# Attention on one core: the large score matmuls move directly behind the transposes, the small ones and the ninth block to the end of the step, and the ninth block into the second transposition bank

## The reference

```python
# q, k, v: (4, 8, 1152, 64)
q_pool = q.reshape(B, H, S // 2, 2, D).mean(axis=3)          # 576 queries of a head
scores = scale * np.matmul(q_pool, k.transpose(0, 1, 3, 2))  # 576 x 1152
scores = scores - np.max(scores, axis=-1, keepdims=True)
attn = np.exp(scores)
attn = attn / (np.sum(attn, axis=-1, keepdims=True) + 1e-09)
x = np.matmul(attn, v)             # then reordered to 2304 tokens x 512
h = x @ w_in                                                 # 512 -> 2048
g = np.maximum(h, 0.0) + alpha * np.minimum(h, 0.0)
return (g @ w_out).astype(np.float32)                        # 2048 -> 512
```

## Time and profile before

| | |
|---|---|
| times of three runs | 1018.55, 1018.21, 1015.3 us; median 1018.21 us |
| profiled execution | 1016.51 us, of which its span is 1014.0 us |
| PE, matmuls | 919.4 us busy (91%), 6896 instructions |
| PE, weight loads | 632.5 us busy (62%) |
| DVE | 528.3 us busy (52%) |
| ACT | 423.4 us busy (42%) |
| POOL | 213.6 us busy (21%) |
| attention stage | until about 596 us |
| network stage | from there, 418 us with PE busy for 409.8 us |

### The profile page before, as it was taken

One profiled execution on the slowest core, in us unless ns is written; L12 is line 12 of the kernel. 1 busy time (PEld: TensorE's weight loads), 2 busy tenths in 40 slices (PEclk: granted clock), 3 DMA queues, 4 the chain that ended last, 5 costly groups with the idle time before them and its releaser, 6 DMA issues. The chain is left out here.

```text
span 1014.0 us, 20768 instructions
## 1 busy us (share of the span) xinstructions
PE 919.4 (91%) x6896; PEld 632.5 (62%) x6896; DVE 528.3 (52%) x836; ACT 423.4 (42%) x963; POOL 213.6 (21%) x182
## 2 busy tenths in 40 slices
PE   3798888889889888888888889999999999999997
PEld 1344444444444444444444459999999999999996
DVE  1456666666666666666666644444444444444442
ACT  1455555555555555555555542222232222322222
POOL 2011112102111111211111023333333333333331
PEclk9899999999999999999999999999999999999999
DMA  7334134224423413532442012122232222422211
GB/s 171 97 77 123 49 75 122 64 57 122 104 63 76 122 47 75 122 87 60 96 121 65 1 32 63 62 62 63 62 125 62 62 63 62 126 63 67 60 48 62
DMA packets 36366, 79.57 MB, mean 78 GB/s; under 512 B 5360, under 2 KB 9456, under 8 KB 36336
## 3 DMA queue, kind: packets, MB, share of 16 engines
q1 hardware_dynamic: 33936, 74.48, 28.4%
q10 hardware_dynamic: 2400, 4.72, 1.3%
HBM read 74.46 MB, written 4.72 MB: 78 GB/s over the span
## 5 line engine op out<-in xcount | busy, mean ns | idle before, releaser
L431 DVE TENSOR_REDUCE neg_max<-s_ps 128x1 f32<-128x1152 f32 x144 | 195.5, 1357 | 111.3 <-DVEq L430 111.3
L529 PE MATMUL s_ps<-k_f,q_f 64*128 64x512 f32 (+1 forms) x640 | 167.6, 657 | 5.2 <-PEq L540 5.2
L570 PE MATMUL pv_ps<-pt,v_f 128*64 128x256 f32 (+1 forms) x1152 | 170.3, 417 | 0.0
L348 ACT ACTIVATE e_sb<-s_ps,neg_max 128x1024 f32<-128x1024 f32 x144 | 160.3, 1113 | 0.0
L341 ACT ACTIVATE e_sb<-s_ps,neg_max 128x128 f32<-128x128 f32 x144 | 53.0, 368 | 221.2 <-ACTq L340 221.1
L570 PEld LDWEIGHTS pv_ps<-pt,v_f 128*64 128x64 f32 x1152 | 71.4, 137 | 112.5 <-issue 82.8
L464 DVE COPY pt<-slot_ps 128x512 f32<-128x512 f32 x144 | 99.5, 691 | 75.6 <-DVEq L463 75.5
L517 PE MATMUL s_ps<-k_end,q_f 128*128 128x128 f32 (+1 forms) x320 | 68.1, 317 | 77.6 <-PEq L591 56.4
L584 PEld LDWEIGHTS slot_ps<-ident,e_sb 64*128 64x128 f32 x2304 | 86.1, 141 | 71.1 <-issue 71.1
L613 PE MATMUL slot_ps<-x_hi,wi_hi 128*128 128x384 f32 x384 | 129.5, 337 | 1.0 <-PEq L609 1.0
L613 PE MATMUL slot_ps<-x_lo,wi_hi 128*128 128x384 f32 x384 | 129.5, 337 | 0.0
(11 more groups left out here) (46 smaller groups left out, 1006.3 us busy)
## 6 DMA issues: line engine op xcount, KB each, us to landing
q_raw<-in_q SPq DMA_DIRECT2D x64, 288.0 KB, 4.6
k_f<-in_k SPq DMA_DIRECT2D x64, 288.0 KB, 4.1
wi_raw<-in_w_in SPq DMA_DIRECT2D x48, 256.0 KB, 2.6
wo_raw<-in_w_out SPq DMA_DIRECT2D x48, 256.0 KB, 2.6
v_f<-in_v SPq DMA_DIRECT2D x32, 288.0 KB, 3.1
out<-pt ACTq DMA_DIRECT2D x6, 768.0 KB, 4.6
k_end<-in_k SPq DMA_DIRECT2D x64, 32.0 KB, 4.0
alpha_sb<-in_alpha SPq DMA_DIRECT2D x1, 8.0 KB, 4.7
```

What stands on the lines that cost most here:

```text
L348: nc.scalar.activation(e_sb[:, b * NKEY + at:b * NKEY + at + n], s_ps[:, S_AT[b] + at:S_AT[b] + at + n], ACT.Exp, bias=neg_max[:, b:b + 1] ...
L431: nc.vector.tensor_reduce(out=neg_max[:, b:b + 1], in_=s_ps[:, S_AT[b]:S_AT[b] + NKEY], op=ALU.max, axis=AX_X, negate=True).then_inc(max_r ...
L529: ins = nc.tensor.matmul(s_ps[to:to + m, S_AT[b] + at:S_AT[b] + at + BANK], q_f[2 * g + h][rows, first:first + m], k_f[2 * g + h][rows, at ...
L570: ins = nc.tensor.matmul(pv_ps[h * D:(h + 1) * D, 0:n], v_f[2 * g + h][:, a, :], pt[:, a, at:at + n], start=(a == 0), stop=(a == KT - 1))
```

## The change

The order of PE's step becomes: transposes of `s`, large scores of `s + 2`, product, ninth block of `s`, small scores of `s + 2`. The ninth block is written into the first 128 columns of `slot_ps[1]`. So it waits for `slot_free[1]`, that is for DVE's copy of slot 1, and the next step's transposes wait for `slot_free[1]` again, which the copy of the ninth block now gives. The semaphore `ninth_free` is gone. The small scores have a semaphore of their own, `s_end_ready`. DVE's row maximum of tile `s + 1` stands at the start of step `s` (the same place in the order of DVE as the end of step `s - 1`), and `scale` moves from the start of t = 0 and t = 5 into t = 8 and t = 4, between the copy of slot 1 and the copy of the ninth block. On ACT the copy of slot 0 comes before the cut.

```diff
--- before.py
+++ after.py
@@ -106,7 +106,7 @@
         BIG = [(0, 512), (128, 640)]
         END = [(1024, 1), (0, 0)]
         BIG_AT = [0, P]
-        NINTH = s_ps[:, 2 * BANK + P:2 * BANK + 2 * P]
+        NINTH = slot_ps[1][:, 0:P]
         y_ps = [[s_ps[:, t * BANK:(t + 1) * BANK] for t in range(3)],
                 [s_ps[:, 3 * BANK:4 * BANK], s_ps[:, 4 * BANK:5 * BANK], pv_ps[:, :]]]
         tail_ps = s_ps[:, 3 * BANK:3 * BANK + 256]
@@ -133,8 +133,8 @@
         exp_done = sem("exp_done")
         tr_ready = [sem(f"tr{i}_ready") for i in range(2)]
         ninth_ready = sem("ninth_ready")
+        s_end_ready = sem("s_end_ready")
         slot_free = [sem(f"slot{i}_free") for i in range(2)]
-        ninth_free = sem("ninth_free")
         inv_ready = sem("inv_ready")
         spread_ready = sem("spread_ready")
         inv_bc_ready = sem("inv_bc_ready")
@@ -351,11 +351,10 @@
 
             def step(s, pair, left=2):
                 t, g = s % TILES, s // TILES % 2
-                if left > 0:
-                    exponential_cut(s + 1)
                 act.wait_ge(tr_ready[0], 1).then_inc(tr_ready[0], -1)
                 nc.scalar.activation(pt_half(t, 0), half_columns(slot_ps[0][:, :]), ACT.Copy).then_inc(slot_free[0], 1)
                 if left > 0:
+                    exponential_cut(s + 1)
                     exponential(s + 1)
                 if t in SPREAD and (t == 6 or pair is not None):
                     n = GROUPS[SPREAD[t]][2]
@@ -427,7 +426,9 @@
         def _(dve):
             def row_max(s):
                 b = s % 2
+
                 dve.wait_ge(s_ready, 2).then_inc(s_ready, -2)
+                dve.wait_ge(s_end_ready, 1).then_inc(s_end_ready, -1)
                 nc.vector.tensor_reduce(out=neg_max[:, b:b + 1], in_=s_ps[:, S_AT[b]:S_AT[b] + NKEY],
                                         op=ALU.max, axis=AX_X, negate=True).then_inc(max_ready, 1)
 
@@ -454,22 +455,22 @@
 
             def step(s, pair, left=2):
                 t, g = s % TILES, s // TILES % 2
-                if t == 0 and pair is not None:
-                    dve.wait_ge(x_sb_free, 1).then_inc(x_sb_free, -1)
-                    scale(0)
-                if t == 5 and pair is not None:
-                    scale(1)
-                    dve.sem_inc(v_free[1 - g], 1)
+                if left > 0:
+                    row_max(s + 1)
                 dve.wait_ge(tr_ready[1], 1).then_inc(tr_ready[1], -1)
                 nc.vector.tensor_copy(pt_half(t, 1), half_columns(slot_ps[1][:, :])).then_inc(slot_free[1], 1)
-                dve.wait_ge(ninth_ready, 1).then_inc(ninth_ready, -1)
-                nc.vector.tensor_copy(pt_ninth(t), ninth_columns(t)).then_inc(ninth_free, 1)
                 if t in INVERT:
                     invert(INVERT[t])
                 if t == 5 and pair is not None:
                     x_high(pair + (0 if s < 2 * TILES else 1))
-                if left > 1:
-                    row_max(s + 2)
+                if t == 4 and s >= TILES:
+                    scale(1)
+                    dve.sem_inc(v_free[1 - g], 1)
+                if t == 8:
+                    dve.wait_ge(x_sb_free, 1).then_inc(x_sb_free, -1)
+                    scale(0)
+                dve.wait_ge(ninth_ready, 1).then_inc(ninth_ready, -1)
+                nc.vector.tensor_copy(pt_ninth(t), ninth_columns(t)).then_inc(slot_free[1], 1)
 
             def unit(f, h):
                 dve.wait_ge(h_ready, 1).then_inc(h_ready, -1)
@@ -490,14 +491,10 @@
                 nc.vector.memset(k_end[i][D:P, :, :], 0.0).then_inc(k_end_zero, 1)
             for i in range(2):
                 dve.sem_inc(slot_free[i], 1)
-            dve.sem_inc(ninth_free, 1)
             dve.sem_inc(pv_free, 1)
             row_max(0)
-            row_max(1)
             over_steps(dve, step)
             dve.wait_ge(alpha_in, 16).then_inc(alpha_in, -16)
-            dve.wait_ge(x_sb_free, 1).then_inc(x_sb_free, -1)
-            scale(0)
             for n in range(PASSES):
                 def hidden(f, i, first, last):
                     unit(f, 0)
@@ -585,15 +582,8 @@
                                                   ident[rows, rows])
                         if a == 2 * CH - 1:
                             ins.then_inc(tr_ready[i], 1)
-
-                pe.wait_ge(ninth_free, 1).then_inc(ninth_free, -1)
-                if left > 0:
-                    pe.wait_ge(exp_cut_done, 1).then_inc(exp_cut_done, -1)
                 if left > 1:
                     begin_scores(s + 2)
-                    small_scores(s + 2)
-                transposed(s, 2 * CH, NINTH).then_inc(ninth_ready, 1)
-                if left > 1:
                     for ins in big_scores(s + 2):
                         ins.then_inc(s_ready, 1)
                 group, tiles = PRODUCT[t]
@@ -602,6 +592,13 @@
                         pe.wait_ge(slot_free[0], 1).then_inc(slot_free[0], -1)
                         spread_inverse(SPREAD[t], slot_ps[0])
                     product(group, g if group == 0 else 1 - g, tiles)
+
+                pe.wait_ge(slot_free[1], 1).then_inc(slot_free[1], -1)
+                transposed(s, 2 * CH, NINTH).then_inc(ninth_ready, 1)
+                if left > 0:
+                    pe.wait_ge(exp_cut_done, 1).then_inc(exp_cut_done, -1)
+                if left > 1:
+                    small_scores(s + 2).then_inc(s_end_ready, 1)
 
             def hidden_unit(n, f, i, h):
                 if h == 0:
@@ -635,20 +632,20 @@
             pe.wait_ge(ident_done, 1).then_inc(ident_done, -1)
             pe.wait_ge(k_end_zero, 4).then_inc(k_end_zero, -4)
             begin_scores(0)
-            small_scores(0)
+            small_scores(0).then_inc(s_end_ready, 1)
             for ins in big_scores(0):
                 ins.then_inc(s_ready, 1)
             begin_scores(1)
-            big_scores(1)
+            for ins in big_scores(1):
+                ins.then_inc(s_ready, 1)
             pe.wait_ge(exp_cut_done, 1).then_inc(exp_cut_done, -1)
-            small_scores(1).then_inc(s_ready, 2)
+            small_scores(1).then_inc(s_end_ready, 1)
             over_steps(pe, step)
 
 
             pe.wait_ge(x_ready, NPAIR - 2)
             hidden_unit(0, 0, 0, 0)
             pe.wait_ge(slot_free[1], 1)
-            pe.wait_ge(ninth_free, 1).then_inc(ninth_free, -1)
             product(1, 1, (0, 1))
             spread_inverse(1, tail_ps)
             product(1, 1, range(2, KT))
```

## The result

The changed kernel takes 993.88 us (runs of 993.28, 993.67 and 994.09; a fourth took 2176.64 us, which nothing here explains, and is left out of the comparison). The kernel before ran once more beside it (1017.14; the median of its four runs is 1017.67). The ratio to it is 0.9768, 95% interval 0.9746 to 0.979: 2.3% faster, where I had forecast 0.6% and a range from 1004 us.

What follows compares the result with a forecast made beforehand. It took the row-maximum-to-large-scores round, elsewhere PE's own work, to bound steps. Steps 6 to 142 +2.1 us, steps 0 to 5 -7.5, the rest 0: -5.4, so 1012 us, range 1004 to 1021.

Steps and rivals of the forecast that it cites:

- The round of before: Kernel before: row maximum, cut, small scores, ninth block, large scores, 3.89 us; binds steps where PE's own work is shorter.
- The tail: Step's end, from ninth block to next transposes: 0.48 to DVE's copy, 0.29 copy, 0.15 semaphore, 0.92 us in sum.
- the long form of the ninth block: The ninth block's matmul, now always behind a product, takes 0.33 us and not 0.27.
- `scale` in the tail: At t = 4 and 8 DVE does `scale` before the ninth block's copy, making ninth block to transposes 1.54 us.
- transposes 0.64 (242.83 to 243.47): Start of each PE step: transposes take 0.64 us to the start of the next row.
- PE's own pieces: PE's work in a step, start to next row: transposes 0.64, large scores 1.06, product 0.58 to 1.77, spread 0.49 or 0.60.
- the sum: Transposes, large scores, spread, product and tail added for t = 0 to 8: 35.99 us a pair, 4.00 a step.
- Steps 0 to 5: First steps, without a product before t = 5: 7.5 us less, between bounds of 5.5 and 9.6.
- my round: Fast first steps without a product: two steps form 0.90 + 3.50 + 0.64 + 1.06 = 6.10 us, 3.05 a step.
- no step can be shorter than 3.48 us: Limit from small scores through row maximum, cut and exponential to the transposes of `s + 1`: 3.48 us a step.
- late small scores: Rival: small scores at the step's end start 0.3 us later, delaying the row maximum; 10 us more, 1022 us; chance 0.17.
- a shorter tail: Rival: the ninth block starts as in its short form, 0.06 us less in seven steps a pair; 1006 us; chance 0.2.

Runs made afterwards that it cites:

- the first run: Changed kernel with the product directly behind the transposes, ahead of the large scores, except at t = 1 and 6: 993.52 us.

## Why the prediction was wrong

- **The round of before** (row maximum, cut, small scores, ninth block, large scores): right. It is gone, and PE waits nowhere from 60 to 540 us for `exp_cut_done`.
- **The tail**: right to 0.02 us, in both forms, the long form of the ninth block and the 0.15 us for the semaphore included. The shortest of its 124 matmuls from 60 to 540 us is 0.327 us. The Trainium skill's rule (TensorE: Matmul & The Clock Gate, Step-by-step: what each phase is for) did not shorten the tail, which is 0.92 us and not 0.86.
- **`scale` in the tail**: right, 1.54 to 1.56, and 8.5 us dearer than at its old place.
- **The step that failed** is the term "transposes 0.64 (242.83 to 243.47)" in PE's own pieces. The row is right, but it is the distance from transposes to *small scores*, which use the full array, and I took it as what transposes cost whatever follows. With the large scores behind them it is 0.52 us. The term stands in all 137 steps from 6 to 142; 15 of them have the large scores of tile 4 behind the transposes (0.65), the last has none: 121 x 0.12 = 14.5 us. The error of that stretch is 14.7 us (forecast 547.8, measured 533.1). The run with the product behind the transposes in four steps and the large scores of tile 4 show that the 0.12 us belong to the neighbour.
- **That 14.5 and 14.7 agree so well is partly luck.** Ahead of `spread_inverse` the large scores take 1.18 to 1.19 us in all 27 cases from 60 to 540 us (216.35 to 217.54), where the sum has 1.06, which is 0.13 us twice a pair, some 4 us. The prediction had the spread find slot 0 free. Now its copy ends at 217.24, 0.30 us ahead of the spread; before, it ended 1.2 us ahead (590.30 and 591.51), and the same two pieces stood 1.06 us apart. So the wait for `slot_free[0]` is the likely cause, but no run tests it. Pieces that came out 0.02 to 0.04 us shorter than in the sum, such as large scores to product (1.02 to 1.05), make up for it.
- I weighed the Trainium skill's rule (TensorE: Matmul & The Clock Gate, Step-by-step: what each phase is for) that weight loads are pulled ahead of matmuls in flight at the ninth block alone, where the load stays exposed. The place where loads did overlap is the one that I had not asked about: the large scores' loads start 0.11 us before those of the transposes end in the changed kernel. The page names as conditions row groups that don't conflict, or a second buffer for the weights. The overlap of the loads agrees with the rule. With the halves exchanged the first load goes to the rows of the last transpose, and it still starts at 205.39, so free row groups alone do not explain the overlap there; the second buffer was not tested.
- **Steps 0 to 5**: the direction was right, the size just outside my bounds: 10.3 instead of at most 9.6 us. PE and ACT at the start of the changed kernel:

```profile
20.77 1.80 PE L526 MATMUL s_ps<-k_f,q_f 64*128 64x512 f32 x4
22.50 0.33 PE L541 MATMUL slot_ps<-ident,e_sb 128*128 128x128 f32 x1
...
23.59 0.72 PE L581 MATMUL slot_ps<-ident,e_sb 64*128 64x64 f32 x16 [0.54 <-PEq L576]
...
26.93 0.72 PE L581 MATMUL slot_ps<-ident,e_sb 64*128 64x64 f32 x16 [0.97 <-PEq L576]
...
27.73 0.60 ACT L355 ACTIVATE pt<-slot_ps 128x512 f32<-128x512 f32 x1 [1.29 <-ACTq L354]
...
28.23 0.36 ACT L341 ACTIVATE e_sb<-s_ps,neg_max 128x128 f32<-128x128 f32 x1
...
30.22 0.71 PE L581 MATMUL slot_ps<-ident,e_sb 64*128 64x64 f32 x16 [0.92 <-PEq L576]
```

The large scores at 20.77 are still slow, 1.73 us to the next row, and the ninth block at 22.50 takes 0.33 us where it took 0.42 on the kernel before; the transposes at 23.59 are 0.72 long, not 1.06. So the matmuls are at their full rate from the second step on, and I had three slow steps. Step 5, too, is 3.70 us long at a granted clock of 1.00, where the kernel before took 7.07 at 0.52, near the lower of the clock's two levels (its window from 43.65 to 50.72 us). In the whole stretch the same 153 matmuls keep PE busy for 15.71 us instead of 23.09, which is 7.4 of the 10.3. The fall to 0.89 of the clock in that stretch did not come back (1.00 in the window), but no run separates how much of the gain is clock and how much is order.

Against that, the fast steps without a product take 3.3 to 3.5 us and not 3.05 (between 23.59 and 36.98 there are four). Here my round left out a link, ACT's copy of slot 0, which the change put ahead of the cut. The row maximum has ended at 27.46, but the cut starts at 28.23, behind the copy: 0.80 us from the transposes to the copy, 0.50 to the cut, 1.99 to the next transposes are the 3.29 us of the step. They also show that "no step can be shorter than 3.48 us" was wrong. The row maximum follows the ninth block's copy on DVE and starts 0.18 us ahead of the transposes in most later steps, not 0.02; the shortest steps there are 3.48 us because of their tails.
- **The rivals**: late small scores did not happen, the row maximum is even earlier than I had it. The time lies below the range because its lower end took in a shorter tail, and not a shorter step ahead of it. (The chance of "faster", 0.66, should have been 0.65 by its own rule.)

## What to carry to other kernels

A distance between two rows belongs to the pair of instructions, not to the first: where a change puts another neighbour behind a piece of work, look for a row with that neighbour. Here the kernel before had none, and then the range has to be wider. Test each part of a reordering by itself. Here one of its moves was worth 73 us, and the moves made along with it cost 51 of them. Two of these were taken back one at a time: the ninth block's bank, which is handed to DVE and back in the last microsecond of a step (8.8 us), and `scale` (8.5 us). And when an experiment's total says "no difference", read its rows: in the first run here a loss and a gain of the same size stood side by side.

## What the runs showed of the hardware

- Sixteen transposes on tiles of 64 rows by 128 columns are followed after 0.52 us (0.51 to 0.55) by matmuls on tiles of the same shape, and after 0.64 to 0.65 us by matmuls that use the full array, 64 columns of it, or tiles of 64 by 64. Which half of the rows comes first makes no difference.
- A full-width transpose behind matmuls that use 64 columns is 0.33 us long (all 124 in the changed kernel from 60 to 540 us), where it is 0.27 behind a full-width matmul.
- From the end of DVE's copy of a bank to PE's next matmul that waited for it, 0.14 to 0.15 us (123 of 124 cases in the changed kernel). From the end of ACT's large exponential to the transposes that waited for it, 0.53 to 0.55 us (76 cases with the ninth block in its own columns); the runs don't say what the longer distance consists of.
